# Moves into x ahead of round 1's decays, weight splits a step sooner, and decay products by level, in an attention and feed-forward kernel

## The reference

```python
for t in range(S):                       # S = 768
    cur = einsum('bhd,bhe->bhde', u * kt, vt)
    y[:, :, t] = einsum('bhd,bhde->bhe', rt, state + cur)
    state = wt[:, :, :, None] * state + einsum('bhd,bhe->bhde', kt, vt)
x = y.transpose(0, 2, 1, 3).reshape(3072, 384)
x = ((x @ w_a) * (x @ w_b)) @ w_out      # gated, 1536 inner columns
h = x @ w_in                             # leaky, 2048 inner columns
out = (maximum(h, 0) + alpha * minimum(h, 0)) @ w_out2
```

## Time and profile before

| | us |
|---|---|
| three runs, median (lowest to highest) | 1035.59 (1034.51 to 1036.74) |
| the profiled execution, its own time | 1035.63 |
| its span, first to last instruction | 1033.6 |
| TensorE busy | 1006.8 (97%) |
| DVE busy | 562.1 (54%) |
| ACT busy | 288.5 (28%) |
| POOL busy | 32.1 (3%) |
| mean granted TensorE clock | 0.993 of full speed |

### The profile page before, as it was taken

One profiled execution on the slowest core, in us unless ns is written; L12 is line 12 of the kernel. 1 busy time (PEld: TensorE's weight loads), 2 busy tenths in 40 slices (PEclk: granted clock), 3 DMA queues, 4 the chain that ended last, 5 costly groups with the idle time before them and its releaser, 6 DMA issues.

```text
span 1033.6 us, 29093 instructions
## 1 busy us (share of the span) xinstructions
PE 1006.8 (97%) x12448; PEld 982.7 (95%) x12448; DVE 562.1 (54%) x1170; ACT 288.5 (28%) x604; POOL 32.1 (3%) x29
## 2 busy tenths in 40 slices
PE   4798999999999999999999999999999999999998
PEld 4798999999999999999999999999999999999998
DVE  7575574664655646646542446655455545555454
ACT  3423413224133142241222433222222222222211
POOL 3500010000000000000000000000000000000000
PEclk9998999999999999999999999999999999999999
DMA  6443331301311113011010222110101010101000
GB/s 182 124 118 96 80 101 29 90 25 29 90 52 46 47 52 91 2 52 37 26 51 9 84 85 85 39 47 1 47 1 47 1 46 0 46 0 46 2 23 23
DMA packets 42168, 53.01 MB, mean 51 GB/s; under 512 B 5185, under 2 KB 42049, under 8 KB 42049
## 3 DMA queue, kind: packets, MB, share of 16 engines
q1 hardware_dynamic: 40144, 50.35, 16.9%
q10 hardware_dynamic: 1904, 0.91, 0.4%
HBM read 39.46 MB, written 9.44 MB: 47 GB/s over the span
## 4 chain that ended last, share of the span: by engine, by line
PE 90%; issue 1%; DVE 1%; ACT 0%; DVEq 0%; ACTq 0%
PE products L166 17%; PE products L167 15%; PE products L168 15%; PE acc L166 11%; PE acc L168 11%; PE acc L167 11%; PE products L702 4%; PE products L746 1%; PE products L717 1%; PE products L731 1%; PE products L679 1%; PE products L762 1%; DVE f_y L926 0%; DVE f_y L920 0%; ACT x_in L513 0%
## 5 line engine op out<-in xcount | busy, mean ns | idle before, releaser
L166 PE MATMUL products<-x_parts,weights_hi 128*128 128x384 f32 x576 | 202.5, 352 | 7.9 <-DVE weights_lo L143 3.3
L167 PE MATMUL products<-x_parts,weights_hi 128*128 128x384 f32 x576 | 195.8, 340 | 0.0
L168 PE MATMUL products<-x_parts,weights_lo 128*128 128x384 f32 x576 | 195.5, 339 | 0.0
L1233 DVE TENSOR_SCALAR leaky_low<-products,leaky_al 128x384 f32<-128x384 f32 x128 | 79.0, 617 | 169.4 <-PE products L168 169.3
L1093 DVE TENSOR_TENSOR g_sb<-a_g,products 128x384 f32<-128x384 f32 x96 | 53.2, 554 | 203.9 <-issue 140.2
L1180 ACT ACTIVATE leaky_g_hi<-leaky_g_sb 128x384 fp32r<-128x384 f32 x128 | 67.3, 525 | 295.0 <-DVE leaky_g_sb L1238 295.0
L513 ACT ACTIVATE g_hi<-g_sb 128x384 fp32r<-128x384 f32 x96 | 50.4, 524 | 257.6 <-DVE g_sb L1093 257.6
L166 PEld LDWEIGHTS products<-x_parts,weights_hi 128*128 128x128 f32 x576 | 109.4, 190 | 12.3 <-issue 5.7
L168 PEld LDWEIGHTS products<-x_parts,weights_lo 128*128 128x128 f32 x576 | 109.5, 190 | 0.0
L167 PEld LDWEIGHTS products<-x_parts,weights_hi 128*128 128x128 f32 x576 | 109.5, 190 | 0.0
L166 PE MATMUL acc<-g_hi,weights_hi 128*128 128x384 f32 x288 | 98.1, 340 | 0.7 <-ACT x_in L513 0.7
(11 more groups left out here) (86 smaller groups left out, 1769.3 us busy)
## 6 DMA issues: line engine op xcount, KB each, us to landing
k_in<-in_k_dram SPq DMA_DIRECT2D x16, 336.0 KB, 4.0
r_in<-in_r_dram SPq DMA_DIRECT2D x16, 336.0 KB, 5.7
stage<-in_w_out_dram SPq DMA_DIRECT2D x14, 384.0 KB, 3.2
w_v<-in_v_dram SPq DMA_DIRECT2D x16, 288.0 KB, 3.8
y_dram<-x_in SPq DMA_DIRECT2D x8, 576.0 KB, 3.2
x_in<-y_dram SPq DMA_DIRECT2D x8, 576.0 KB, 4.4
out_dram<-leaky_out_sb SPq DMA_DIRECT2D x7, 576.0 KB, 3.3
stage<-in_w_dram SPq DMA_DIRECT2D x10, 336.0 KB, 3.8
```

The costliest lines, as they stand in the source:

```text
L166: pe.matmul(out, w_hi, x_hi, start=first, stop=False)
L167: pe.matmul(out, w_hi, x_lo, start=False, stop=False)
L168: return pe.matmul(out, w_lo, x_hi, start=False, stop=last)
L1233: dve.tensor_scalar(self.low[f % 2][:, :], h, 0.0, self.al[:, f:f + 1], ALU.min, ALU.mult).then_inc(self.low_ready, 1)
```

## The change

- `products_of_w` takes a list of levels. In round 0 each stream makes its first level alone; the level after it is one instruction for both streams, made after both merges of level 1; the other four, also for both streams, follow the key step of level 2 on stream 0. The key step of level 1 on stream 1 stands right after that stream's leaf merge. `f_count` counts the new order.
- Round 1's decays are issued by SP after the moves of round 0 (phase 10), and no longer by ACT between its output copies.
- `EARLY` is 5: piece 5 is loaded at step 11, behind the moves, not at step 9; its halves are made in slot f=0, by ACT and DVE, not by ACT and POOL at step 11. `FIRST_NEW` gives slots 0 to 6 pieces 5 | 6 | 7, 8 | 9 | 10 | 11, 12 | 13, 14 and slot 7 piece 15; before they were none | 6 | 7 | 8 | 9 | 10, 11 | 12, 13 and 14, 15. A load of a piece in tile 0 is tied to the split of the piece three before it, and moves with it.

```diff
-EARLY = 6
+EARLY = 5
-HI_AT = [2, 3, 4, BEFORE_TILES, 11, 11]
+HI_AT = [2, 3, 4, BEFORE_TILES, 11]
-LO_AT = [7, 8, 9, 9, 11, 11]
-LOAD_AT = [7, 8, 9, 11, 11, 11]
+LO_AT = [7, 8, 9, 9, 11]
+LOAD_AT = [7, 8, 11, 11, 11]
-FIRST_NEW = [6, 6, 7, 8, 9, 10, 12, 14, 16, 17, 18, 18, 18]
+FIRST_NEW = [5, 6, 7, 9, 10, 11, 13, 15, 16, 17, 18, 18, 18]
 def f_count(duo, index, j):
-    return index + 1 + (6 * j if duo == 0 else 6 * (duo + 1))
+    if duo == 0:
+        return j + 1 if index == 0 else index + 2
+    return 6 * duo + index + 2
...
                     elif phase == 10:
                         move_last_unit(n)
-                        if 1 < n + 1 < STAGED_FROM:
+                        if n + 1 < STAGED_FROM:
                             load_w(n + 1, 0)
                             load_w(n + 1, 1)
...
                         if n == 0:
-                            load_first_w(0)
                             shared.split_hi(act, BETWEEN_OUTPUTS)
-                            load_first_w(1)
                         copy_outputs(n, 1)
...
                 first_step_k(0, 0)
-                products_of_w(0, 0, 1)
+                products_of_w(0, 0, 1, (1,))
                 dve.wait_ge(leaf_mask_loaded, 32)
                 dve.wait_ge(cleared, 1)
                 merge_leaf(0, 0)
                 step_k(0, 0, 1)
                 first_step_k(0, 1)
-                products_of_w(0, 1, 1, (True, False))
+                products_of_w(0, 1, 1, (1,))
                 merge_leaf(0, 1)
-                products_of_w(0, 1, 1, (False, True))
-                for step in range(BEFORE_TILES):
-                    if step != 2:
+                step_k(0, 1, 1)
+                merge_level(0, 0, 1)
+                merge_level(0, 1, 1)
+                products_of_w(0, 0, 2, (2,))
+                step_k(0, 0, 2)
+                products_of_w(0, 0, 2, range(3, 7))
+                for step in range(3, BEFORE_TILES):
+                    if step > 3:
                         attend_early(step)
                     attend(step)
```

More of the change, by code:

```diff
@@ L564, in copy_outputs @@
                             copy(hi, ps).then_inc(copied, 1)
-                def load_first_w(j):
-                    act.wait_ge(products_done[j], after(0, 8))
-                    load(act, w_v, w, 1, j, TT, TT, w_loaded[j], into=S * j)
                 def attend(step):
@@ L907, in _, with products_of_w @@
             def _(dve):
-                def products_of_w(n, first, streams, parts=(True, True)):
+                def products_of_w(n, first, streams, levels):
                     def of(tile, at, step, count):
@@ L913, in products_of_w @@
                     w_tile = decays_of(n)
[L915 to L926, removed]
+                    for level in levels:
+                        h = 1 << level
+                        if level == 1:
+                            if n > 0:
+                                wait_moved(dve, n)
+                            for j in range(first, first + streams):
+                                dve.wait_ge(w_loaded[j], 16 * (n + 1))
+                            source, at = w_tile, 0
+                        else:
+                            dve.wait_ge(f_done, f_count(n, level - 2, first + streams - 1))
+                            source, at = f_y, F_AT[h // 2]
+                        dve.tensor_tensor(of(f_y, F_AT[h], 1, S // h), of(source, at, 2, S // h), of(source, at + 1, 2, S // h),
                                           ALU.mult).then_inc(f_done, 1)
@@ L1043, in attend @@
                     elif phase == 1 and n > 0:
-                        products_of_w(n, 0, 2)
+                        products_of_w(n, 0, 2, range(1, 7))
                     elif 2 <= phase <= 5:
```

## The result

The changed kernel takes 1025.82 us (median, 1024.64 to 1027.71) against 1036.16 for the kernel before on the same chips. The ratio is 0.9904, with a 95% interval of 0.9883 to 0.9924, so it is 8 to 12 us faster. Timed twice more it gave 1026.40 (ratio 0.9917, 0.9903 to 0.9931) and 1025.81 (0.9907, 0.9891 to 0.9924). I had forecast 1028.1, with 1026.5 as the lower end: the right direction and the right places, but too small. Its profiled execution took 1026.15 us, 9.5 less than that of the kernel before.

A forecast was written before the change was run, and what follows sets the result against it. TensorE, busy 97% of the span, was taken as the bound, with its costly waits before 96 us. Gains of 6.2 (splits sooner) and 1.3 us (front) sum to 7.5: 1035.6 to 1028.1 us, range 1026.5 to 1031.9.

The forecast's parts named there:

- Part 1: Weight splits one slot sooner remove TensorE's wait before block 6 (3.3 us) and the half clock behind it (2.9): 6.2 us.
- the 4.6 us named there: The forecast gain, instead of 7.5 us, for runs where the clock's fall would have missed the stall before block 6.
- Part 2: Round 0's decay products made by level, so DVE's key steps come sooner: the front is 0.6 us ahead, bounds 0 and 1.5.
- Three POOL steps fall among these DVE operations: In round 0's levels, POOL's steps delay DVE's queue; TensorE starts level 3 of stream 1 at 22.05 against 22.64.
- so the 0.6 stays to the moves: Later levels of round 0 have the same operations, so the front's 0.6 us lead lasts until the moves into x.
- Parts 2 and 3: Decay products by level, plus moves into x ahead of decays and piece 5: 1.3 us together, set by DVE's queue.
- The last low part, which ends at 46.08, 45.5 then: End of round 0's attention outputs, after which x's thirds 1 and 2 can be issued: 45.5 us instead of 46.08.
- The decays now go out behind the moves on SP: 48.3 now, 47.75 with the front's lead: SP issues round 1's decay loads after the moves, at 47.75 us and 48.2; they land at 52.5 and 53.2.
- Rival (a): New idle time around the first gated products lowers the clock, costing 3.4 us: gain 4.1, 1031.5 us; chance 0.20.
- (b): The front gives nothing, as POOL's steps fall badly and late decays put DVE's queue 1 us later: 1029.7 us; chance 0.11.
- (c): Slower than before, as late decay loads hold DVE's queue and delay g_lo of block 0: say 1038 us; chance 0.03.
- (d): The wait on the low half moves to slot 2, where DVE has two halves; 1.3 us left, 1034.3 us; chance 0.04.

The follow-up runs named there:

- part 2 alone: The kernel before with only round 0's decay products made by level: 1033.84 us against 1035.50, ratio 0.9985 (0.9975 to 0.9996).
- part 1 alone: The kernel before with only FIRST_NEW changed, pieces 8 to 14 split a step sooner, EARLY still 6: 1030.63 us against 1035.50, ratio 0.9958.
- the changed kernel without part 1: The changed kernel with FIRST_NEW of the kernel before from block 2 on: 1030.44 us, ratio 0.9966 (0.9949 to 0.9984).
- the trace with the decays ahead: The changed kernel with round 1's decays issued by ACT ahead of the moves again: median 1026.77 us, ratio 0.9913; the traced run took 1029.08.

## Why the prediction was wrong

**Part 1: right in place; right in size for the profiled pair only, by luck of the trace.** 6.2 forecast, 6.03 in the traces. But the trace of before had the long fall of the clock behind the wait, 6.8 us. The five others with the wait unfilled had 3.4 us, and there part 1 is worth 4.6 to 4.9. Undone in the changed kernel it costs about 5 us, and alone it gave 3 to 6. The wait itself was 3.2 to 3.7 us each time. The clock's part is 2.6 us in the pair of traces, 1.3 to 1.6 in the others. In 65 timed executions of the kernel before with a mean clock of 0.993, 0.995 or 0.997, the medians are 1036.0 (20 executions, with one of 0.992), 1035.0 (25) and 1034.1 (20). The profiled one was among the 0.993 and has 13.7 us at 0.50 in its two falls; the trace of part 2 alone has 0.995 and 10.2 us, that of part 1 alone 0.997 and 6.8. So each step is about 3.4 us more at 0.50, and costs about 1 us. This agrees with the sentence on the clock gate from the Trainium skill ("TensorE: Matmul & The Clock Gate"), which the trace of before couldn't show: how long the clock stays low after the same wait differs from run to run. It did not take all of the clock's part out of the sum, as in the 4.6 us named there, because a fall behind the wait appeared in every trace in which the wait was left unfilled; in five of six it took some 1.3 us.

**Part 2: forecast 0.6, found in no trace by the end of the levels.** "Three POOL steps fall among these DVE operations" was right in kind, and in part 2 alone level 3 of stream 1 started at 22.00, where I had 22.05. What failed is *"so the 0.6 stays to the moves"*: the keys were turned from 30.43 there and from 30.46 before. In the changed kernel the third of the POOL steps made DVE's key step end at 22.6 instead of 21.95; this was the lower bound of 0. What part 2 gives for certain lies outside the span, 0.2 to 0.3 us, and my sum had no term for it. The times of part 2 alone allow more, unexplained.

**Parts 2 and 3, forecast 1.3, gave 3.15 in the pair: this is the step that failed.** It is no accident of one trace: in the times the changed kernel without part 1, which is these two parts, is 3.5 us (1.7 to 5.3) faster than the kernel before. The order of the links was right. Two terms were sized wrong, and of the 1.9 us by which down of block 1 came sooner than forecast in the pair, the first makes 1.4 and the chain behind it 0.5.
- *"The last low part, which ends at 46.08, 45.5 then".* I took the time at which the attention ends from one trace as if the kernel set it. It doesn't: the clock rises somewhere from 39.4 to 45.0 us, and the end moved from 43.65 to 46.79 with it (and with waits for nothing that the profile shows, as in the changed kernel's second trace). The trace of before had a late rise. In the old order that mattered little, as the first product started at 48.9 to 50.4 in the four traces with the moves' wait unfilled, with ends at 43.65 to 46.08 and no order between the two. In the new order it is passed on: the lead at g_sb of block 5 was 3.15, 1.84 and 3.45 in the three traces of the changed kernel. So the change opened a gain that depends on when the attention ends in a run, and I had sized it from a run in which it ended late.
- *"The decays now go out behind the moves on SP: 48.3 now, 47.75 with the front's lead".* I let SP take 2.25 us from the last low part to its next issue, as in the trace of before. It took 1.4 in nine of ten traces with the new order of loads and 2.0 in the tenth. But it also took 1.4 in three of the six with the old order, so this too was a number that moves between runs. In the pair next to nothing of it was left when the second load of decays landed, as this took 5.6 us and not the 5.0 I gave it, and the 0.5 us of the chain come from DVE's work behind it; in the other two traces of the changed kernel that landing was 0.8 and 1.1 us sooner than I had it, counted from the last low part.

**Rival (a), a fall of the clock in the new idle time, at 0.20, did not come.** The wait for g_lo was 1.0 us or missing and not 2, the waits for the moves 0.5 to 2.0 in sum, and in all timed runs of the changed kernel the mean clock was 1.000. TensorE's wait of 2.8 us did let it fall in the trace with the decays ahead. (b) named DVE's queue rightly as the bound, but expected it to cost time and not to leave a gain; (c) and (d) didn't occur. What I should have asked of the bounds is which numbers of the one trace another run could move. The upper bound on the front was 2.7, below the 3.15 of the pair, and a rise of the clock 4 us sooner alone brings 2.

## What to carry to other kernels

When a chain has two feeders, one timed by compute and one by DMA, a single trace shows only the later one as binding; ask how far the other one moves between runs before sizing what a reordering gives. In this kernel a long wait of TensorE had two prices, its length and the clock behind it, and filling it with products of no use measures the second by itself in a few lines. When a load is put off, look for every split or copy that waits on it in another engine's queue, and what stands behind that: twice here (piece 5, piece 8) it was ACT's copy for the next gated product.

## What the runs showed of the hardware that I had not expected

- More work made the kernel faster: 34 products of no use took the kernel before from 1035.1 to 1030.9 us.
- SP was through with its last two moves, issued while ACT issued two, 1.4 us after the last low part in 9 of 10 traces with the new order of loads, but 1.4 to 2.3 us after it in the six with the old order. One trace doesn't give this price.
- DVE's key step took 1.13 us where it started 0.3 us behind a step of POOL, and 0.56 where it started just ahead of it.
- The low clock behind the same wait of 3.2 to 3.7 us lasted 3.4 us in five traces and 6.8 in one.
- Moves of 48 KB issued at the same place took 4.5 and 5.0 us to land with the decays and piece 5 ahead, and in the trace of part 1 alone TensorE started on them 6.7 us after SP's first issue.
